# Preparing the decays of a gated linear attention anew: lines of 16 with carries, three full head groups, earlier start, unrolled tiles

## The chip, the cores and the metric

The kernel runs on one core of a Trainium2 chip. The metric is the device time of one execution in microseconds (us), median of the timed runs. The engines are TensorE (PE), VectorE (DVE), ScalarE (ACT), GpSimd (POOL) and SyncE (SP), which here only issues DMAs.

## The reference, cut to what matters

Three layers follow each other: an attention with complex decays, a SoLU expert layer, and a top-2 mixture of 8 experts. The change touches only how the decays of the first layer are prepared.

```python
# q, k, v, a_re, a_im: batch 4, heads 8, positions 768, head_dim 48
mag = np.sqrt(a_re * a_re + a_im * a_im)
scale = np.minimum(mag, 0.999) / (mag + 1e-06)
a_re_n, a_im_n = (a_re * scale, a_im * scale)
for t in range(S):
    ar, ai = (a_re_n[:, :, t, :, None], a_im_n[:, :, t, :, None])
    new_re = ar * S_re - ai * S_im
    new_im = ar * S_im + ai * S_re
    kv = np.einsum('bhd,bhe->bhde', k[:, :, t], v[:, :, t])
    S_re, S_im = (new_re + kv, new_im)
    y[:, :, t] = np.einsum('bhd,bhde->bhe', q[:, :, t], S_re)
```

Then x = y as 3072 tokens of 384; h = x @ w_in (384 to 1024); SoLU, layer norm and @ w_out (1024 to 384); router logits, top 2 of 8, and for each expert relu(x @ w1) @ w2.

## The kernel before

**Two phases.** The first phase goes over 24 tiles of 128 positions (batch b = 0..3, chunk c = 0..5, tile n = 6b + c) and ends with tokens scattered to their experts' regions in HBM. The second goes over 31 slots of 256 tokens, and the gathers write the output. The diff leaves the second phase alone, but for a renamed constant.

**Decays in a tile.** Positions of a chunk are referred to its middle. For each position the kernel holds the running complex product F of the decays from the middle outwards and 1/|F|^2. Query and key are weighed by these (`weigh`, the positions of one half each) and multiplied by F (`qp` on VectorE, `kp` on GpSimd), so that scores are plain matmuls. The state between chunks is multiplied by the "state decays" `md`.

**The preparation of a batch**, before: head pairs on 2 x 48 of the 128 partitions, 4 pairs x 6 chunks x 128 positions = 3072 elements a partition, in three pieces. Loads (`load_a`); squares (ScalarE), `m2` (GpSimd), four ScalarE passes `logs`, `zsum` (GpSimd), `scale` (ScalarE), normalising (`norm` on GpSimd, `norm_im` on VectorE), `neg` (ScalarE). Then `products_start` and the running product, `product_op`: 63 steps of three VectorE instructions of 96 elements, one position outwards on both sides of all 24 middles at a time. Then `state_decays` (8 small ones), squares, `f2`, Ln and Exp, `newton` (GpSimd), `inverses` (VectorE), and `publish` (ScalarE copies F to a second buffer). In batch 0 all this is ahead of the tiles. Batch b + 1 is prepared inside batch b: the product steps in chunks 2, 3 and 4, as `fill()` between other VectorE work; squares and logs in chunks 0 and 1, the inverse in 5.

**The tiles are software-pipelined.** In iteration n each engine works on m = n - 1 (attention), i = n - 2 (first matmul, SoLU), j = n - 3 (second matmul) and g_ = n - 4 (router), in an order written out by hand; semaphores tie the engines. TensorE: transposes of kp(m) (L1247), first half of the hidden matmuls (i) (L1285, waits for xl), score matmuls (m) interleaved with the second half (L1305, wait for qp and zl), the state product w(m) with the second matmul (j) (L1345, L1326), y(m) (L1359, L1361), logits (L1376), transposes of z(i) (L1247). y(m) goes through ScalarE's xh (L802) and VectorE's xl (L1132) to the hidden matmuls of the next iteration. VectorE's last instructions in an iteration are xl(m) and then q_products(n) (L982); GpSimd's `weigh` (L505, L507) is first and `kp` (L515) comes behind the masking of at(m) (L536), before the state products. ScalarE: zh(j) (L722), kt, wide, softplus, at(m) (L759), exp, x2, centring, x2t, xh(m). Chunks 0 to 5 of batches 0 and 3 are unrolled, batches 1 and 2 are a hardware loop whose body is six chunks.

Of the kernel before, what the change touches and what calls it, by code (L numbers as in the profile page):

```python
# [15 lines left out]
P = 128  # L16
# [7 lines left out]
F = 1024  # L24
# [11 lines left out]
PIECES = 3  # L36
CP = C // PIECES
# [38 lines left out]
def solu_moe_program(nc, q, k, v, a_re, a_im, w_in, w_out, g_ln, w_gate, w_noise, noise, w1, w2, out):  # L76
# [3 lines left out]
    with ExitStack() as ctx:  # L80
# [22 lines left out]
        ar = m1("ar", [P, NP, C, P])  # L103
        m1_ai = m1.at
        ai = m1("ai", [P, 2, NP, C, P])
        fw = m1("fw", [P, 2, NP, C, P])
        early_end = m1.at
        fu = m1("fu", [P, 2, NP, C, P])
        rc = m1("rc", [P, NP, C, P])
# [14 lines left out]
        ct1 = m1("ct1", [P, 2, G, 2])  # L124
        ct2 = m1("ct2", [P, 2, G, 2])
        hd = [m1(f"hd{i}", [P, 2, NP, C]) for i in range(3)]
        ud = [m1(f"ud{i}", [P, 2, NP, C - 1]) for i in range(2)]
        md = m1("md", [P, 3, NP, C - 1])
        mdn = m1("mdn", [P, 3, NP, C - 1])
        xh = m1("xh", [P, NP, P], F32R)  # L130
        xl = m1("xl", [P, NP, P], F32R)
        z = m1("z", [P, F])
# [56 lines left out]
        NG = 4  # L189
        m3 = Map(nc, tables_end)  # L190
        ga = [m3(f"ga{i}", [P, 2, DM]) for i in range(NG)]
        gb = [m3(f"gb{i}", [P, DM]) for i in range(NG)]
        gc = [m3(f"gc{i}", [P, DM]) for i in range(NG)]
# [10 lines left out]
        md_ready = sem("md_ready")  # L204
# [5 lines left out]
        a_re_loaded = sem("a_re_loaded")  # L210
        a_im_loaded = sem("a_im_loaded")
# [7 lines left out]
        an_re = sem("an_re")  # L219
        an_im = sem("an_im")  # L220
# [6 lines left out]
        nt_step = sem("nt_step")  # L227
        rc_done = sem("rc_done")
        pub_done = sem("pub_done")
# [58 lines left out]
        g_loaded = [sem(f"g_loaded{i}") for i in range(NG)]  # L288
        first_done = sem("first_done")
        both_done = sem("both_done")  # L290
        out_sent = [sem(f"out_sent{i}") for i in range(NG)]
# [6 lines left out]
        CUM = 4 + 3 * (HALF - 1)  # L298
        block = ctx.enter_context(nc.Block())

        def piece(t, g):
            return t[:, :, g * CP:(g + 1) * CP, :]

        def slot_piece(t, s, g):
            return t[:, s, :, g * CP:(g + 1) * CP, :]

        STEPS = {0: 0, 1: 0, 2: 19, 3: 22, 4: 22, 5: 0}
        assert sum(STEPS.values()) == HALF - 1
# [1187 lines left out]
```

## Time and profile before

| | us |
|---|---|
| timed runs, median (lowest to highest) of 3 | 1587.64 (1586.15 to 1588.35) |
| span of the profiled execution | 1599.5 |
| busy in it: TensorE / VectorE / ScalarE / GpSimd | 1197.5 / 1032.7 / 720.5 / 470.9 |
| mean granted TensorE clock | 0.890 of full speed |

The profiled execution has no time of its own beside its span, which lies 12 us above the median of the timed runs. A sum made from the profile is made against the 1599.5. The clock column of the profile is 1.0 at 2.4 GHz and 0.5 at 1.2 GHz.

### The profile page before, as it was taken

The numbers are of one execution on the slowest core, as the hardware profiler recorded it, in microseconds if no ns is written. First come the engines' busy times: TensorE is split into PE (matmuls) and PEld (weight loads), VectorE is DVE, ScalarE is ACT, GpSimd is POOL, SyncE is SP. The second block draws the span as 40 slices with busy tenths as digits, with TensorE's granted clock in tenths as the row PEclk, the third lists the DMA queues.
The fourth block names the chain that finished last, engine by engine and source line by source line (L and its number), as shares of the span: only waits on it lengthen the run. The fifth ranks groups of instructions, "written<-read, shape, count | busy, mean of one in ns | idle before, by whom it ended". The sixth has DMA issues, their size and how long they took to land.

```text
span 1599.5 us, 24940 instructions
## 1 busy us (share of the span) xinstructions
PE 1197.5 (75%) x8058; PEld 1026.0 (64%) x8058; DVE 1032.7 (65%) x2193; ACT 720.5 (45%) x1094; POOL 470.9 (29%) x378
## 2 busy tenths in 40 slices
PE   0001448888888778789999827999999999999920
PEld 0001336666666556556777627999999999999910
DVE  2896299867998569984444335666666666666523
ACT  5305622657226662254334314555555555555500
POOL 4204633467435664445345110000000000000056
PEclk9999668878888878987999958999999999999965
DMA  8103100041000401001111037666666566656357
GB/s 161 68 0 58 31 16 16 26 84 46 31 26 26 97 19 45 25 26 35 41 50 41 21 138 247 215 219 211 237 206 231 199 234 216 230 202 223 131 154 211
DMA packets 78718, 179.64 MB, mean 112 GB/s; under 512 B 7344, under 2 KB 46384, under 8 KB 77872
## 3 DMA queue, kind: packets, MB, share of 16 engines
q1 hardware_dynamic: 68032, 147.60, 29.5%
q0 software_dynamic: 6144, 18.88, 4.0%
q10 hardware_dynamic: 4464, 12.19, 1.9%
q8 instruction: 40, 0.66, 0.2%
q14 instruction: 38, 0.31, 0.1%
HBM read 146.01 MB, written 32.64 MB: 112 GB/s over the span
## 4 chain that ended last, share of the span: by engine, by line
PE 51%; DVE 20%; issue 10%; POOL 7%; DMA 5%; ACT 4%; SPq 2%; DVEq 0%; POOLq 0%; ACTq 0%
PE bank L1431 17%; PE bank L1256 16%; DVE fw L937 5%; DVE ct L934 5%; PE bank L1285 4%; PE bank L1326 4%; DVE ct L930 4%; PE bank L1247 3%; POOL ga L613 2%; DMA ai<-in_a_im 2%; PE bank L1305 2%; PE bank L1359 1%; POOL ar L489 1%; PE bank L1345 1%; POOL ai L495 1%
## 5 line engine op out<-in xcount | busy, mean ns | idle before, releaser
L613 POOL DMA_INDIRECT ga<-ys,row_u x48 | 45.9, 957 | 605.1 <-DMA ys<-yo 590.7
L1256 PE MATMUL bank<-sxh,w1h 128*128 128x256 f32 x744 | 212.3, 285 | 1.9 <-DVE sxl L1209 1.9
L1256 PE MATMUL bank<-sxh,w1l 128*128 128x256 f32 x744 | 210.3, 283 | 0.0
L1256 PE MATMUL bank<-sxl,w1h 128*128 128x256 f32 x744 | 210.2, 283 | 0.0
L858 ACT ACTIVATE hh<-bank 128x256 fp32r<-128x256 f32 x248 | 95.2, 384 | 218.7 <-PE bank L1256 218.7
L1221 DVE SCALAR_TENSOR_TENSOR hl<-bank,hh 128x256 fp32r<-128x256 f32 x248 | 104.8, 423 | 129.4 <-ACT hh L858 129.3
L1431 PE MATMUL bank<-w2h,hh 128*128 128x384 f32 x496 | 170.4, 344 | 6.1 <-DVE hl L1221 3.2
L1431 PE MATMUL bank<-w2l,hh 128*128 128x384 f32 x496 | 166.9, 336 | 0.0
L1431 PE MATMUL bank<-w2h,hl 128*128 128x384 f32 x496 | 166.7, 336 | 0.0
L1198 DVE TENSOR_TENSOR w1l<-raw,w1h 128x1024 fp32r<-128x1024 f32 x93 | 113.9, 1226 | 52.8 <-ACT w1h L822 52.8
L1247 PE MATMUL bank<-ident,kp 128*128 128x128 f32 x192 | 33.4, 333 | 151.4 <-POOL kp L515 149.7
L1256 PEld LDWEIGHTS bank<-sxh,w1h 128*128 128x128 f32 x744 | 140.8, 189 | 2.3 <-DVE sxl L1209 2.3
L1256 PEld LDWEIGHTS bank<-sxh,w1l 128*128 128x128 f32 x744 | 141.8, 191 | 0.0
L1256 PEld LDWEIGHTS bank<-sxl,w1h 128*128 128x128 f32 x744 | 141.3, 190 | 0.0
L1204 DVE TENSOR_TENSOR w2l<-raw,w2h 128x768 fp32r<-128x768 f32 x124 | 118.6, 958 | 30.9 <-ACT w2h L827 30.9
L1247 PEld LDWEIGHTS bank<-ident,kp 128*128 128x128 f32 x192 | 29.6, 177 | 151.8 <-issue 151.8
L930 DVE TENSOR_TENSOR ct<-fw,ar 128x96 f32<-128x96 f32 x252 | 104.1, 413 | 7.6
L822 ACT ACTIVATE w1h<-raw 128x1024 fp32r<-128x1024 f32 x93 | 97.7, 1052 | 19.7 <-DMA raw<-in_w 19.7
L827 ACT ACTIVATE w2h<-raw 128x768 fp32r<-128x768 f32 x124 | 103.6, 838 | 3.2 <-DMA raw<-in_w 3.2
L1431 PEld LDWEIGHTS bank<-w2h,hh 128*128 128x128 f32 x496 | 94.3, 190 | 12.1 <-issue 8.4
L934 DVE TENSOR_TENSOR ct<-fw,ai 128x96 f32<-128x96 f32 x252 | 101.1, 401 | 0.0
L937 DVE TENSOR_TENSOR fw<-ct,ct 128x96 f32<-128x96 f32 x252 | 93.6, 372 | 6.8
(182 smaller groups left out, 2920.1 us busy)
## 6 DMA issues: line engine op xcount, KB each, us to landing
raw<-in_w SPq DMA_DIRECT2D x62, 1536.0 KB, 6.7
xg<-xs SPq DMA_DIRECT2D x31, 384.0 KB, 7.1
ys<-yo ACTq DMA_DIRECT2D x31, 384.0 KB, 6.4
ar<-in_a_re SPq DMA_DIRECT2D x8, 576.0 KB, 8.2
ai<-in_a_im SPq DMA_DIRECT2D x8, 576.0 KB, 14.7
qk<-in_q SPq DMA_DIRECT2D x48, 96.0 KB
qk<-in_k SPq DMA_DIRECT2D x48, 96.0 KB
vt<-in_v SPq DMA_DIRECT2D x24, 192.0 KB, 2.4
```

Source lines behind the costliest of these rows:

```text
L822: nc.scalar.activation(w1h[par][:, cc, :], raw1[:, cc, :], ACT.Copy).then_inc(w1_hi, 1)
L827: nc.scalar.activation(w2h[par][:, W2C * j:W2C * (j + 1), :], raw2[:, W2C * j:W2C * (j + 1), :], ACT.Copy).then_inc(w2_hi, 1)
L858: nc.scalar.activation(hh[:, f % NH, :], bank[:, f % 2, 0:CAP], ACT.Relu).then_inc(hh_done, 1)
L930: V.tensor_tensor(ct1[:], fwg[:, :, :, prev], arg[:, :, :, step].to_broadcast([P, 2, G, 2]), ALU.mult).then_inc(cum_step, 1)
L934: V.tensor_tensor(ct2[:], fwg[:, ::-1, :, prev], aig[:, :, :, step], ALU.mult).then_inc(cum_step, 1)
L937: V.tensor_tensor(fwg[:, :, :, new], ct1[:], ct2[:], ALU.add).then_inc(cum_step, 1)
L1198: V.tensor_tensor(w1l[par][:, cc, :], raw1[:, cc, :], w1h[par][:, cc, :].bitcast(F32), ALU.subtract).then_inc(w1_lo, 1)
L1204: V.tensor_tensor(w2l[par][:, cut, :], raw2[:, cut, :], w2h[par][:, cut, :].bitcast(F32), ALU.subtract).then_inc(w2_lo, 1)
L1221: V.scalar_tensor_tensor(out=hl[:, f % NH, :], in0=bank[:, f % 2, 0:CAP], scalar=0.0, in1=hh[:, f % NH, :].bitcast(F32), op0=ALU.max, op1= ...
L1247: ins = nc.tensor.transpose(out_, in_, ident[:])
L1256: ins = MM(dst, stationary[a_](cc), moving[b_](cc), start=(n_ == 0), stop=(n_ == len(terms) - 1))
L1431: ins = MM(bank[:, 2 + u, 0:DM], a_[:, f % NH, rows], b_[par][:, f, :], start=(f == 0 and k_ == 0), stop=(f == FC - 1 and k_ == 2))
```

## The change

- **Layout.** The eight heads of 48 rows are packed into three groups that fill all 128 partitions (`by_lane` on the host): six heads as before, the other two, in strips of 16 rows, in the 16 rows that each pair left free. A partition has 2304 elements. The first half of each chunk is stored in reversed order. After the products, SyncE copies the strips to a fourth group (`spread_cum` 12 DMAs, `spread_md` 6, `spread_rc` 6 for each range).
- **Products.** Lines of 16 positions at a time (15 steps of three instructions, 288 elements for a whole batch), then three carries: a line is multiplied by the last element of the line before (6 instructions of 576 elements).
- **Ranges.** Batch 0 is prepared in two ranges, chunks 0 and 1 ahead of the tiles, chunks 2 to 5 behind VectorE's work of tiles 0 and 1. The others are one range each, in two parts. `PREP` says in which chunk what stands; the load of a batch can start once `newton` of the batch before has ended.
- **Engines.** `weigh` goes from GpSimd to VectorE, into q_products, behind xl. `norm` and `newton` go to VectorE, the second as two fused instructions. qp and kp become two instructions each, one for each half. `publish` goes; F has two buffers by batch.
- **Order of the start.** No memsets ahead of the first load; the low parts of the weights (`weights_rest`) are made after the query product of tile 0.
- **Unrolling.** All 24 tiles and the four that drain the pipeline are unrolled.

```diff
+RANGES = ((0, 0, 2), (0, 2, C), (1, 0, C), (2, 0, C), (3, 0, C))
+PARTS = ((0, 0, 0, 2), (1, 0, 2, 4), (1, 0, 4, 6), (2, 1, 0, 3), (2, 1, 3, 6),
+         (3, 2, 0, 3), (3, 2, 3, 6), (4, 3, 0, 3), (4, 3, 3, 6))
...
+        PREP = {0: {"load": 2, "logs": 2, "scale": 3, "chain": (4, 5), "decays": 5, "early": None, "late": 5, "post": 5}}
+        for b_ in range(1, B - 1):
+            PREP[b_] = {"load": 0, "logs": 0, "scale": 1, "chain": (2, 3, 4), "decays": 4, "early": 5, "late": None, "post": 5}
...
-            for c in range(C):
-                body(0, c, c, True)
-            with eng.Fori(1, B - 1) as b:
-                for c in range(C):
-                    body(b, c, b * C + c, True)
-            for c in range(C):
-                body(B - 1, c, (B - 1) * C + c, False)
+            for n in range(T):
+                body(n // C, n % C, n, n < T - C)
```

GpSimd (its `k_products`, and what leaves its list):

```diff
-                nc.gpsimd.tensor_tensor(qk[:, 0, :, 0:HALF], qk[:, 0, :, 0:HALF], rc[:, :, c, 0:HALF],
-                                        ALU.mult).then_inc(qkw_done, 1)
-                nc.gpsimd.tensor_tensor(qk[:, 1, :, HALF:P], qk[:, 1, :, HALF:P], rc[:, :, c, HALF:P],
-                                        ALU.mult).then_inc(qkw_done, 1)
...
-                wait(pool, pub_done, PIECES * b + c // CP + 1)
+                pool.wait_ge(qkw_done, 2 * (n + 1))
                 wait(pool, a_mm, n)
...
+                for h_ in range(2):
+                    cols = slice(HALF * h_, HALF * (h_ + 1))
+                    cum = cums[b % 2][:, :, :, 1, c, :] if h_ else cums[b % 2][:, :, :, 0, c, ::-1]
+                    nc.gpsimd.tensor_tensor(kp[:, :, :, cols], cum, qk[:, 1:2, :, cols].to_broadcast([P, 2, NP, HALF]),
+                                            ALU.mult).then_inc(kp_done, 1)
```

SyncE, in the body of a tile:

```diff
+                if when(b, c, "load"):
+                    load_a(b + 2)
...
+                if when(b, c, "decays"):
+                    spread_cum(b + 2)
+                    spread_md(b + 2)
+                if more and c == 5:
+                    spread_rc(b + 2)
```

ScalarE, in the body of a tile: the first three stand before at(m), `scale` of the second part behind exp, the rest behind xh(m).

```diff
+                if when(b, c, "logs"):
+                    act.wait_ge(w_ready, 2)
+                    act.wait_ge(gaps_ready, 6)
+                    squares(2 * b + 3)
+                    squares(2 * b + 4)
+                if when(b, c, "scale"):
+                    logs(2 * b + 4)
+                    scale(2 * b + 3)
+                if when(b, c, "early"):
+                    inverse_squares(2 * b + 3)
+                    inverse_squares(2 * b + 4)
...
+                if when(b, c, "logs"):
+                    logs(2 * b + 3)
+                if when(b, c, "scale"):
+                    neg(2 * b + 3)
+                    neg(2 * b + 4)
+                if when(b, c, "late"):
+                    inverse_squares(2 * b + 3)
+                    inverse_squares(2 * b + 4)
+                if when(b, c, "post"):
+                    inverse(2 * b + 3)
+                    inverse(2 * b + 4)
```

VectorE:

```diff
+                if k < CHAIN:
+                    v, step = k // 3 + 1, k % 3
...
+                    if step == 0:
+                        dve.wait_ge(cum_step, at0)
+                        V.tensor_tensor(t1, cum[:, :, :, :, v - 1],
+                                        blocks(ar, r)[:, :, :, v].unsqueeze(1).to_broadcast([P, 2, 2 * NG, nu]),
+                                        ALU.mult).then_inc(cum_step, 1)
...
+            def q_products(b, c, n):
+                r = b + 1 if n >= 2 else 0
+                dve.wait_ge(qk_loaded, 64 * (n + 1))
+                dve.wait_ge(rc_spread, 96 * (r + 1))
+                dve.wait_ge(rc_done, PARTS_UPTO[r])
+                V.tensor_tensor(qk[:, 0, :, 0:HALF], qk[:, 0, :, 0:HALF], rc[:, :, 0, c, ::-1], ALU.mult).then_inc(qkw_done, 1)
+                V.tensor_tensor(qk[:, 1, :, HALF:P], qk[:, 1, :, HALF:P], rc[:, :, 1, c, :], ALU.mult).then_inc(qkw_done, 1)
...
                 if has(n):
                     q_products(b, c, n)
+                if when(b, c, "scale"):
+                    norm(2 * b + 3)
+                    norm(2 * b + 4)
+                if when(b, c, "decays"):
+                    state_decays(b + 2)
+                if when(b, c, "post"):
+                    f2(2 * b + 3)
+                    f2(2 * b + 4)
+                    newton(2 * b + 3)
+                    newton(2 * b + 4)
+                if n == 0:
+                    weights_rest(0)
+                    weights_rest(1)
+                    norm(1)
+                    norm(2)
+                    products_start(1)
+                    for k_ in range(CHAIN):
+                        product_op(1, k_)
```

TensorE waits for w_ready before the first hidden matmul instead of ahead of everything; its order is the same.

## Rows read from the trace of the kernel before

**Rows 1.** Page: busy time of each engine (span 1599.5 us); the chain by engine.

```profile
PE 1197.5 (75%) x8058; PEld 1026.0 (64%) x8058; DVE 1032.7 (65%) x2193; ACT 720.5 (45%) x1094; POOL 470.9 (29%) x378
...
PE 51%; DVE 20%; issue 10%; POOL 7%; DMA 5%; ACT 4%; SPq 2%; DVEq 0%; POOLq 0%; ACTq 0%
```

**Rows 2.** Stages: start:end length, busy us (instructions) by engine, granted clock, DMA share, GB/s.

```profile
0.00:145.60 145.60, 0.00 (x0) 0.00 (x0) 102.50 (x228) 50.96 (x48) 42.52 (x31) 1.00 0.29 63
...
180.80:230.90 50.10, 20.12 (x136) 14.93 (x136) 38.83 (x76) 24.86 (x34) 26.14 (x17) 0.66 0.04 12
...
323.40:358.30 34.90, 28.07 (x164) 20.05 (x162) 20.47 (x36) 21.31 (x27) 22.10 (x17) 0.76 0.48 96
358.30:391.70 33.40, 28.90 (x188) 22.27 (x186) 22.10 (x37) 26.95 (x37) 24.22 (x14) 0.89 0.11 31
391.70:427.05 35.35, 28.60 (x170) 21.15 (x171) 33.51 (x95) 10.92 (x20) 18.80 (x17) 0.81 0.11 34
427.05:461.40 34.35, 27.41 (x175) 20.56 (x174) 32.99 (x100) 9.09 (x17) 12.58 (x12) 0.85 0.09 30
...
521.40:555.60 34.20, 27.49 (x177) 19.85 (x178) 19.63 (x37) 21.40 (x27) 22.63 (x16) 0.85 0.51 99
...
724.90:760.00 35.10, 32.67 (x165) 23.35 (x165) 13.70 (x37) 14.53 (x19) 18.27 (x16) 0.66 0.12 40
760.00:877.30 117.30, 117.30 (x867) 86.88 (x866) 56.39 (x162) 45.08 (x80) 53.61 (x53) 1.00 0.13 41
```

**Rows 3.** Timeline (start us, length us), boundary of tile 19, and one wait at 329.

```profile
329.81 1.23 PE L1305 MATMUL bank<-qp,kp 64*128 64x128 f32 x8 [3.30 <-DVE zl L1024]
...
781.73 0.43 PE L1361 MATMUL bank<-at,vt 128*48 128x128 f32 x4
782.20 0.60 ACT L802 ACTIVATE xh<-bank 112x512 fp32r<-112x512 f32 x1 [0.85 <-PE bank L1361]
782.83 0.69 DVE L1132 TENSOR_TENSOR xl<-bank,xh 112x512 fp32r<-112x512 f32 x1 [1.64 <-ACT xh L802]
783.44 1.22 DVE L982 TENSOR_TENSOR qp<-fu,qk 128x1024 f32<-128x1024 f32 x1
783.68 1.04 PE L1247 MATMUL bank<-ident,kp 128*128 128x128 f32 x8
```

**Rows 4.** Windows of TensorE alone in a chain tile: length, busy, clock.

```profile
447.20:452.10 4.90, 0.00 (x0) 0.90 0.00 0
...
454.20:461.30 7.10, 5.87 (x30) 0.50 0.09 31
```

**Rows 5.** Timeline of VectorE: a full-size product, and product steps.

```profile
50.35 3.48 DVE L962 TENSOR_TENSOR ai<-ai,fw 128x1024 f32<-128x1024 f32 x3
...
56.79 0.35 DVE L930 TENSOR_TENSOR ct<-fw,ar 128x96 f32<-128x96 f32 x1
57.05 0.35 DVE L934 TENSOR_TENSOR ct<-fw,ai 128x96 f32<-128x96 f32 x1
...
57.79 0.35 DVE L930 TENSOR_TENSOR ct<-fw,ar 128x96 f32<-128x96 f32 x1
```

**Rows 6.** GpSimd's kp beside a VectorE product (timeline); a ScalarE pass (groups).

```profile
439.60 2.46 POOL L515 TENSOR_TENSOR kp<-fu,qk 128x1024 f32<-128x1024 f32 x1
439.73 2.53 DVE L934 TENSOR_TENSOR ct<-fw,ai 128x96 f32<-128x96 f32 x1
...
L641 ACT ACTIVATE fw<-fw 128x1024 f32<-128x1024 f32 x12 | 12.7, 1059 | 0.4
```

**Rows 7.** Loads: the start, the decays of batch 1, expert weights (page).

```profile
39.35 11.08 DVE L896 TENSOR_SCALAR raw_out<-raw_out,g_sb 128x384 f32<-128x384 f32 x8 [27.52 <-DMA nz<-in_noise]
...
145.88 0.80 SPq L363 DMA_DIRECT2D ar<-in_a_re  x2
162.75 1.06 ACT L631 ACTIVATE fw<-ai 128x1024 f32<-128x1024 f32 x1 [3.92 <-DMA ai<-in_a_im]
...
raw<-in_w SPq DMA_DIRECT2D x62, 1536.0 KB, 6.7
```

More of the change, by code:

```diff
@@ L529, in body @@
-                filling = static and n == 1
-                if more and c == 1 and not filling:
-                    zsum(b + 1, 0)
-                    zsum(b + 1, 1)
+                has = lambda t: 0 <= t < T
                 if has(m):
@@ L688, in _, with neg @@
[L688 to L697 removed]
+            def neg(q):
+                act.wait_ge(an_done, 3 * (q + 1))
+                nc.scalar.activation(part(an, q), part(ai, q), ACT.Copy, scale=-1.0).then_inc(neg_done, 1)
@@ L699, in _ @@
+            act.wait_ge(tiny_ready, 2)
+            squares(0)
+            logs(0)
+            scale(0)
+            neg(0)
+            for q in (1, 2):
+                squares(q)
+            for q in (1, 2):
+                logs(q)
+            for q in (1, 2):
+                scale(q)
             act.wait_ge(raw_loaded, 48)
@@ L702, in _ @@
             nc.scalar.activation(wo_hi[:], raw_out[:], ACT.Copy).then_inc(w_hi_ready, 1)
[L703 to L709 removed]
+            inverse_squares(0)
+            inverse(0)
+            for q in (1, 2):
+                neg(q)
             def body(b, c, n, more):
[L712 removed]
                 m, i, j, g_ = n - 1, n - 2, n - 3, n - 4
[L714 to L718 removed]
+                has = lambda t: 0 <= t < T
                 if has(j):
@@ L792, in body @@
                                          accum_out=mv[c % 2][:, 2:3]).then_inc(var_done, 1)
-                if more and c == 1 and not filling:
-                    prepare(b, (scale, 0), (scale, 1), (scale, 2))
                 if has(j):
@@ new lines, in norm @@
+            def norm(q):
+                _, _, c0, c1 = PARTS[q]
+                s_ = cum_part(q, 0)
+                dve.wait_ge(sc_done, q + 1)
+                V.tensor_tensor(part(ar, q), part(ar, q), s_, ALU.mult).then_inc(an_done, 1)
+                halves = [t.rearrange("p (g h) x -> p g h x", h=2) for t in (part(ai, q), s_)]
+                low, high = ([t[:, :, h_, :] for t in halves] for h_ in range(2))
+                V.scalar_tensor_tensor(out=low[0], in0=low[0], scalar=-1.0, in1=low[1], op0=ALU.mult,
+                                       op1=ALU.mult).then_inc(an_done, 1)
+                V.tensor_tensor(high[0], high[0], high[1], ALU.mult).then_inc(an_done, 1)
@@ L1001, in body @@
                 m, i, j, g_ = n - 1, n - 2, n - 3, n - 4
-                has = lambda t: not static or 0 <= t < T
-                made = [3 * sum(STEPS[x] for x in range(c))]
-                share = made[0] + 3 * STEPS[c] if more else made[0]
+                has = lambda t: 0 <= t < T
+                chain = PREP[b]["chain"] if more else ()
+                total = CHAIN + CARRY
+                upto = lambda k: total * k // len(chain)
+                made, share = ([upto(chain.index(c))], upto(chain.index(c) + 1)) if c in chain else ([0], 0)
@@ L1058, in body @@
                     V.tensor_tensor(hot[:, 2, :], hot[:, 0, :], hot[:, 1, :], ALU.add).then_inc(gate_step, 1)
-                if more and c == 5:
-                    for g in range(PIECES):
-                        f2(b + 1, g)
-                filling = static and n == 1
-                fill(share - 20 - made[0])
+                fill(share - 8 - made[0])
                 if has(i):
@@ L1125, in body @@
                 fill(share - made[0])
-                if more and c == 1 and not filling:
-                    for g in range(PIECES):
-                        norm_im(b + 1, g)
                 if has(m):
```

628 lines of the change are left out of this document (308 added, 320 removed).

## The prediction

> **What bounds the kernel now.** I read the header and the chain first, then the span cut into stages, then the instructions at one tile boundary, and last the durations. The header and the chain [rows 1] say that TensorE is busy 75% of 1599.5 us and carries half of the chain; VectorE has 20% of it. Where each holds is read from the stages [rows 2]. I cut the first phase at q(n), the start of the query product (L982) of tile n; "body c" is the stretch that ends at the q of chunk c of its batch. Four regimes are to be seen. Until q(0) at 145.6 us TensorE does nothing and VectorE is busy for 102.5 us: the decays of batch 0 are a serial preparation. Tiles 0 and 1 are slow too (q(2) at 230.9). In the batches that prepare the next one a tile takes 33 to 39 us, and in the chain tiles (427.05 to 461.40) VectorE is busy for 33.0 of 34.35 us, so VectorE sets them. In batch 3, with nothing left to prepare, five tiles take 117.3 us, 23.46 each, with TensorE busy all the time at the full clock: that is TensorE's floor. There VectorE is busy for only 11.3 us a tile. The expert slots and the gathers behind them are the same code in both kernels; I leave them alone.
>
> **The change, part by part: the element work.** The prices of VectorE come from two rows [rows 5]: instructions of 96 elements follow each other at 0.26 us, and three of 1024 take 3.48, so one of n elements costs about 0.17 us + 0.97 ns x n, and a step of three with its two waits (1.00 us for 96 elements) costs 0.22 us above three times that. Before, a batch has 63 steps, 63 us. After, it has 15 steps of 288-element instructions, 3 x 0.45 + 0.22 = 1.56 us each, 23.4 in all, and 3 carries of six 576-element instructions, 6 x 0.73 + 0.22 = 4.6 us each, 13.8 in all: 37 us instead of 63. VectorE also gets scaling (5.4 us a batch), f2 2.6, Newton 5.1 and, in every tile, two weighings of 256 elements (0.83 us). Its sum per batch falls, and the chain tiles need 11.3 + 0.8 + 10.9 (seven steps) = 23 us, or 27.5 for the one with the carries. VectorE is no longer the bound there. What goes away on ScalarE (publish, three-part neg) and GpSimd (weigh, norm, Newton) is off the path once these engines have idle time; their share of VectorE's blocking is in the 23 us already.
> The row shows instructions of 96 elements at 0.26 us [rows 5]. The Trainium skill, VectorE: DVE Perf Modes, section The TRN2 errata, has 58 + n cycles in its table, 0.16 us for 96 elements, and says itself that the measured fixed part is nearer 150 cycles. By the table the preparation of batch 0 would be some 11 us shorter still, and my time 11 us lower; the trace agrees with the 150.
>
> **The start.** VectorE's first long wait ends when the last small load lands, at 39.35 [rows 7]. Only a third of the decays (0.8 instead of 2.4 MB) is ahead of it now: 28 us (26 to 33). Scaling w_out, norm, neg and start: 36. Chain of 96 elements, 15 x 1.00 = 15, with the four GpSimd sums of parts 1 and 2 in its way (7 us): 58. Carries 3 x 2.3: 65. Decays, squares, f2, logarithm and exponential, Newton, all serial: 71.5. Then SyncE issues 24 spreading DMAs at 0.4 us each [rows 7], most of them while that goes on, and the last land about 78: q(0), against 145.6. Behind it VectorE does in program order weights_rest 7.8, norm 4, start 1.2 and 15 steps of 192 elements (19.2), plus GpSimd's products: q(1) at 119.5, against 180.8. After that the carries, decays, f2 and Newton of the second range run until 145.5; only then may the load of batch 1 start. A pair of such loads takes 16.9 us from issue to landing [rows 7]; in rows of 128 partitions it may do as well as a weight load (1.5 MB in 6.7 us), so 10 to 16. ScalarE waits for both loads before it evacuates at(1), and q(2) follows y(1): 174, against 230.9. So the start gains 57 us.
>
> **What a tile costs then.** At a floor boundary [rows 3] y ends at 782.16, xh runs to 782.80, xl starts at 782.83, the query product at 783.44, and TensorE starts the transposes of kp at 783.68 with no wait, because GpSimd had made kp in the middle of the tile. After the change VectorE weighs q and k itself, and does so behind xl. GpSimd's kp can start only then, and TensorE's next instruction in order is the transpose of kp. From 783.44: 0.83 for the weighings, then two halves of kp (2.46 us for the whole, so 1.2 each) and two halves of the query product (0.65 each) that exclude each other: a VectorE product of 0.35 us lasts 2.53 while kp runs [rows 6]. kp is ready 3.3 (GpSimd first) to 4.5 us after TensorE wants it. Behind kp in GpSimd's queue stand the state products, the scatter and rstd; their readers (wide about 8 us into the tile, x2 about 20) come later. The load of the next q and k waits for kp too, and has 20 us of cover. Nothing is charged for these. So TensorE gets a gap of 3.3 to 4.5 us in every tile, and the floor becomes 23.46 + 4.0 = 27.5. The clock comes on top: in the 4.9 us gap from 447.20 the granted clock falls, and it is 0.50, the 1.2 GHz level, until 461.30 [rows 4]: 9.1 us at half speed behind the gap, in which at most 4.5 us of work are lost. Bounds 0 and 4.5; the work behind the new gap is denser than there, so I take the middle, 2.5, and 30 us a tile; with the gap's own bounds a tile lies between 26.8 and 32.5.
> The Trainium skill, TensorE: Matmul & The Clock Gate, section HAM oscillation, speaks against this change in the same way: a wait repeated in each iteration lets each one start at the lower clock. By full clock throughout, the five last tiles would give back 12 us of what I charge.
>
> **The preparation around the boundaries.** ScalarE's zh of the next tile stands behind the preparation of this one, and zl and the score products wait for it; one such wait of 3.30 us is there already [rows 3]. Its instructions of 1024 elements take 1.06 us [rows 6], those of 1152 some 1.2. Body 1: squares are summed by GpSimd only behind kp, so logs (4 x 1.25) end 11.7 us after the weighing, zl 2.2 later, and TensorE wants it at 8: 30 + 6 = 36. Body 2: norm of both parts on VectorE, interleaved with GpSimd's state products, ends at 11.8, neg at 13, then start and four fills stand ahead of zl: ready at 17.4, so 40. Bodies 3, 4, 5: 30, 31, 30. Body 0: f2, ScalarE's inverse and Newton end at 13.9, zl is 15.3; the load is issued behind the six rc spreads at 16.6, lands after 10 to 16 us, and all four squares stand ahead of at: 43 (40 to 47). Body 0 of batch 3 has no load: 37.5.
>
> **The sum**, beside before [rows 2]: bodies 3, 4, 5 of batch 0 (36, 40, 37, two chain shares of 19 us each) give q(5) at 287 against 323.4; body 0, 45: q(6) at 332 against 358.3. Batch 1: 167 and 43: q(12) at 542 against 555.6. Batch 2: 167 and 37.5: q(18) at 746.5 against 760.0. Batch 3: 5 x 30 = 150: q(23) at 896.5 against 877.3, and kp(23) is later by 4: +23. At 27.5 a tile it is +11. I take +15. The profiled execution spans 1599.5, so the changed one spans about 1614; it lies 12 above the median of the timed runs (1587.64), and on their footing the forecast is 1603. Unrolling I cost at nothing: batch 3 is unrolled before as well, and TensorE is never idle in it. The looped tiles leave VectorE idle for 1.4 us of 34.35 [rows 2], so the most that registers can cost is 12 x 1.4 = 17 us; what sets these tiles afterwards is kp, so none of it is taken.
>
> **Rivals.** (1) Faster: the stalls of zl at the boundaries do not come about, because the ScalarE and VectorE work there fits into the gap that kp opens anyway. For it: kp's gap ends 4 us into the tile and only what is later than 8 us costs. Price: 6 in body 1, 10 in body 2, 7 in body 0, three times: up to 69, likely two thirds, 46: 1603 - 46 = 1557. It decides from 15 us on, that is from a fifth of the price. (2) The gap at kp isn't there or is under 1 us (if GpSimd's halves overlapped VectorE): 9 tiles that TensorE bounds win 6 us, 54: 1549; rows 6 speak against it. (3) The start's gain is given back to the last microsecond: 1587 +- 3. (4) Worse: the loads land late as well and the clock stays low for two thirds of each tile: 20 tiles x 1.5 + 3 x 4 = 42 more, 1645. (5) The page's VectorE table holds: 1592.
>
> **Chances and range.** Slower as forecast or by (4): 0.56, of it (4) 0.08. Rival (1) 0.28, (2) 0.06, (5) and other small gains 0.04: faster 0.38. Within 0.2% (3 us, about what a measurement can tell from no change): 0.06. The range 1560 to 1635 leaves out the upper part of (4) and the lower parts of (1) and (2). The likeliest case's own range is 1592 to 1625.
>
> **What would show it.** Right: q(0) near 78, q(2) near 174; in the last five tiles of the first phase a period near 30, a wait of TensorE's kp transposes for GpSimd of 3.3 to 4.5 us in each, and a granted clock below 1 where it was 1.00; score products that wait for zl in bodies 0, 1 and 2. Wrong: a period of 24 there, or batches 1 and 2 well under 200 us, or a start that ends after 100 us.

## The result, and the profile after

| | before | after |
|---|---|---|
| timed runs, median (lowest to highest), us | 1587.99 (1586.15 to 1592.81), 4 runs | 1605.95 (1603.61 to 1606.88), 4 runs |
| span of the profiled execution | 1599.5 | 1603.5 |
| mean granted TensorE clock | 0.890 | 0.880 |

The changed kernel is slower, by 1.1%: the ratio is 1.0107, with a 95% interval of 1.0086 to 1.0129. The forecast was 1603 us and slower.

The page of the kernel after, busy time of the engines and the chain by engine, answers to [rows 1]:

```profile
PE 1203.9 (75%) x8058; PEld 1031.3 (64%) x8058; DVE 919.7 (57%) x1864; ACT 659.5 (41%) x1022; POOL 380.3 (24%) x316
...
PE 53%; issue 18%; DVE 9%; POOL 7%; SPq 4%; ACT 4%; DMA 3%; POOLq 0%; ACTq 0%; DVEq 0%
```

VectorE lost 113 us of work and fell from 20% to 9% of the chain; GpSimd lost 91, ScalarE 61. The time did not follow. The windows of the kernel after, cut at q(n) like [rows 2] and with the same columns, say where it stayed:

```profile
0.00:73.40 73.40, 0.00 (x0) 0.00 (x0) 40.55 (x102) 28.70 (x29) 15.69 (x23) 1.00 0.48 129
112.82:165.47 52.65, 21.41 (x136) 15.64 (x136) 25.82 (x46) 17.16 (x22) 10.18 (x6) 0.61 0.21 68
277.24:321.18 43.94, 32.27 (x181) 23.27 (x179) 22.58 (x51) 20.68 (x27) 12.21 (x10) 0.74 0.32 97
321.18:359.17 37.99, 31.10 (x173) 22.69 (x173) 9.99 (x36) 20.48 (x26) 17.80 (x11) 0.78 0.08 26
359.17:394.55 35.38, 25.58 (x173) 18.95 (x173) 30.67 (x71) 11.80 (x19) 16.61 (x10) 0.86 0.10 29
...
424.46:454.83 30.37, 25.97 (x173) 19.24 (x173) 26.77 (x58) 9.37 (x17) 13.19 (x10) 0.89 0.11 33
485.23:523.79 38.56, 28.66 (x173) 20.73 (x173) 20.39 (x42) 18.01 (x24) 16.66 (x10) 0.82 0.29 95
686.49:722.85 36.36, 26.93 (x173) 19.85 (x173) 20.38 (x43) 13.90 (x21) 16.65 (x10) 0.86 0.14 36
722.85:872.24 149.39, 129.64 (x865) 96.09 (x865) 49.52 (x177) 45.76 (x81) 47.18 (x47) 0.91 0.11 35
```

The last row is the clearest. Five tiles of batch 3, which prepare nothing, took 117.30 us at the full clock in [rows 2]; now they take 149.39 with the same matmuls. By stages, from these rows and the starts of the query product that lie between them:

| stretch | before | after | difference |
|---|---|---|---|
| to q(2) | 230.9 | 165.5 | -65.4 |
| q(2) to q(5) | 91.6 | 111.8 | +20.2 |
| q(5) to q(11) | 198.9 | 208.0 | +9.1 |
| q(11) to q(17) | 203.5 | 201.3 | -2.3 |
| q(17) to q(18) | 35.0 | 36.4 | +1.3 |
| q(18) to q(23) | 117.3 | 149.4 | +32.1 |
| behind q(23) | 722.2 | 731.3 | +9.0 |

They sum to +4.0, the difference of the two spans; the medians differ by 18.0. The last of the experiments shows where the other 14 are. The timeline of the kernel after at the last tile boundary (start us, length us) answers to [rows 3]:

```profile
870.34 0.60 ACT L802 ACTIVATE xh<-bank 112x512 fp32r<-112x512 f32 x1 [0.85 <-PE bank L1413]
870.40 0.35 SPq L427 DMA_DIRECT2D vt<-in_v  x1
870.91 1.07 PE L1300 MATMUL bank<-ident,z 128*128 128x128 f32 x8
870.96 0.69 DVE L1172 TENSOR_TENSOR xl<-bank,xh 112x512 fp32r<-112x512 f32 x1 [3.16 <-ACT xh L802]
871.57 0.41 DVE L1030 TENSOR_TENSOR qk<-qk,rc 128x256 f32<-128x256 f32 x1
871.90 0.42 DVE L1031 TENSOR_TENSOR qk<-qk,rc 128x256 f32<-128x256 f32 x1
...
872.24 1.28 DVE L1038 TENSOR_TENSOR qp<-cum,qk 128x512 f32<-128x512 f32 x2
872.41 3.47 POOL L557 TENSOR_TENSOR kp<-cum,qk 128x512 f32<-128x512 f32 x2 [11.95 <-DVE qk L1031]
...
875.93 0.90 PE L1300 MATMUL bank<-ident,kp 128*128 128x128 f32 x3 [3.95 <-POOL kp L557]
```

Read upwards from the last row: TensorE has done the transposes of z and then idles 3.95 us for kp; kp began 0.09 us after the second weighing ended; the weighing stands behind xl; and GpSimd had idled for 11.95 us before it. The data was there, only the order was not. The view of waits (TensorE, 60 to 900 us; total, times, longest) says it for all tiles:

```profile
PE bank L1300 <- POOL kp L557: 214.7, 24, 88.4
PE bank L1411 <- POOL at L575: 24.7, 3, 20.8
PE bank L1357 <- DVE zl L1076: 23.4, 8, 6.6
```

The longest, 88.4, is the start, and so are the 19.1 us of the tile after it. The other 22 are one in each tile, 107.2 us together. They are not equally long: 3.95 where nothing is prepared, 6.5 in bodies 0 of batches 2 and 3, and 9.16 in bodies 2. The timeline of the boundary into body 2 of batch 1 (GpSimd's kp, VectorE's normalising, TensorE):

```profile
359.34 8.69 POOL L557 TENSOR_TENSOR kp<-cum,qk 128x512 f32<-128x512 f32 x2 [9.31 <-DVE qk L1031]
...
360.38 1.35 DVE L1002 TENSOR_TENSOR ar<-ar,cum 128x1152 f32<-128x1152 f32 x1
...
364.92 0.75 DVE L1007 TENSOR_TENSOR turn_a<-turn_a,cum 128x576 f32<-128x576 f32 x1
...
368.08 1.97 PE L1300 MATMUL bank<-ident,kp 128*128 128x128 f32 x8 [9.16 <-POOL kp L557]
```

VectorE's products stand back to back from 359.17 to 365.67, 6.5 us, at their usual pace; kp takes 2.50 us in the middle of a tile of the kernel with early weighing (below), and 8.69 here, about the sum of both. GpSimd gets only what VectorE leaves here.

### The profile page after: what moved, and what is told of

It is laid out like the page before. It is cut to its first block, busy times and chain, and to the rows that moved or that the text cites. A ratio compares the mean times of both kernels' runs of the same rounds, so it can differ in the third digit from the quotient of the medians.

```text
span 1603.5 us, 23562 instructions
## 1 busy us (share of the span) xinstructions
PE 1203.9 (75%) x8058; PEld 1031.3 (64%) x8058; DVE 919.7 (57%) x1864; ACT 659.5 (41%) x1022; POOL 380.3 (24%) x316
## 3 DMA queue, kind: packets, MB, share of 16 engines
q1 hardware_dynamic: 75424, 151.17, 28.9%
## 4 chain that ended last, share of the span: by engine, by line
PE 53%; issue 18%; DVE 9%; POOL 7%; SPq 4%; ACT 4%; DMA 3%; POOLq 0%; ACTq 0%; DVEq 0%
PE bank L1483 17%; PE bank L1309 16%; PE bank L1336 8%; PE bank L1357 3%; PE bank L1300 3%; POOL ga L647 3%; PE bank L1378 2%; POOL kp L557 2%; DMA turn_a<-in_a_im 2%; SPq L395 1%; POOL at L575 1%; PE bank L1411 1%; ACT at L765 1%; DVE ct L939 1%; DVE cum L949 1%
## 5 line engine op out<-in xcount | busy, mean ns | idle before, releaser
L1300 PE MATMUL bank<-ident,kp 128*128 128x128 f32 x192 | 46.8, 425 | 214.7 <-POOL kp L557 214.7
L1300 PEld LDWEIGHTS bank<-ident,kp 128*128 128x128 f32 x192 | 37.3, 222 | 220.4 <-POOL kp L557 132.1
L557 POOL TENSOR_TENSOR kp<-cum,qk 128x512 f32<-128x512 f32 x48 | 110.1, 2313 | 265.4 <-DVE qk L1031 265.4
L1336 PE MATMUL bank<-wi_hi,xh 112*128 112x512 f32 x192 | 99.6, 519 | 0.0
L1357 PEld LDWEIGHTS bank<-qp,kp 64*128 64x128 f32 x768 | 57.4, 208 | 60.3 <-issue 60.3
```

The lines of the kernel that those rows point to most:

```text
L557: nc.gpsimd.tensor_tensor(kp[:, :, :, cols], cum, qk[:, 1:2, :, cols].to_broadcast([P, 2, NP, HALF]), ALU.mult).then_inc(kp_done, 1)
L1300: ins = nc.tensor.transpose(out_, in_, ident[:])
L1336: ins = MM(bank[:, 4 + half, :], (xh, xl)[a_][0:PR, cc, :], (wi_hi, wi_lo)[b_][0:PR, cc, 512 * half:512 * half + 512], start=(k_ % (3 * NP ...
L1357: ins = MM(bank[:, 2 + h_, p_ * P:(p_ + 1) * P], kp[r_, s, p_, :], qp[r_, s, p_, :], start=(s == 0), stop=(s == 1))
```

## The experiments

Where q(n) is given for a kernel, it is the start of its query product. "The kernel before" in each ratio was timed on the same chip. My theory: the wait for kp, made by weighing behind xl, costs each tile its gap and then a stretch at the lower clock. Rivals: the half-size products or something else in the new code is slow wherever it stands; the preparation at the boundaries is what counts; the gap is dear only because TensorE has nothing else in it.

**Weighing earlier.** VectorE weighs q and k of the next tile in the middle of this one, ahead of the maximum for the SoLU, instead of behind xl; GpSimd also waits for the copied strips.

```diff
+                if has(n):
+                    weigh(b, c, n)
...
                 if has(n):
                     q_products(b, c, n)
```

> The changed kernel with the weighing of q and k moved in VectorE's order from behind xl to the middle of the tile (ahead of nmax), so that GpSimd makes kp behind the mask of at, as before the change. Theory A (kp, chained behind xl, is what lengthens every tile): the 3.95 us gap of TensorE at the kp transposes is gone, the five last tiles take 23.7 us instead of 29.9 with the clock at 1.00, the tiles of chunks 3 to 5 in batches 1 and 2 some 25.5 instead of 30.4, body 0 and 1 some 2 to 3 us less each; in all about 95 us less than the changed kernel: 1511 us. Rival B (the preparation work at the boundaries and VectorE's fuller list set the tiles, and kp only waits where something else is late anyway): under 30 us less, 1576 or more, and the last tiles stay above 28.

Measured: 1499.11 us (1493.78 to 1507.95), ratio 0.9432 (0.9368 to 0.9496), 107 us below the changed kernel and 12 below what I expected. The windows of the first body of batch 3 and of the five tiles after it:

```profile
616.18:658.82 42.64, 34.96 (x175) 25.19 (x174) 17.54 (x42) 13.56 (x20) 10.71 (x10) 0.64 0.12 36
658.82:775.92 117.10, 117.10 (x867) 86.67 (x866) 57.92 (x176) 45.07 (x80) 47.37 (x48) 1.00 0.13 41
```

The five tiles are back at the floor, 23.42 each, so the half-size kp costs nothing where it isn't waited for. Two rows of this kernel's timeline at such a boundary, beside the 3.95 us above:

```profile
728.42 1.07 PE L1307 MATMUL bank<-ident,z 128*128 128x128 f32 x8
...
729.33 1.04 PE L1307 MATMUL bank<-ident,kp 128*128 128x128 f32 x8
```

It is the one position of two instructions that turns a kernel 1% slower than before into one 5.7% faster. What is left above the floor is now in the waits for zl:

```profile
PE bank L1364 <- DVE zl L1081: 56.4, 13, 8.5
```

They were 23.4 in 8 before the edit: part of what kp's wait had covered now shows itself, in bodies 0 (37.9 to 42.6 us) and 2 (34.7 and 34.9). Body 0 of batch 3, 36.4 us before the edit, even takes 42.6, at a clock of 0.64; body 0 of batch 2 has the same wait of 7.68 us and takes 37.9 at 0.82.

**The wait alone, in the kernel before.** GpSimd's kp waits for xl in all chunks but 1; nothing else of the change is in.

```diff
+                if c != 1:
+                    apart(pool, (xt_lo, n))
```

> The kernel before the change with one wait more: GpSimd's kp of a tile waits for xl of the tile before (in chunks 0, 2, 3, 4, 5; in chunk 1 it would deadlock). Its decays, layout and loops are those of before. Theory A: TensorE gets a gap of 3.0 to 3.6 us at the kp transposes and the lower clock behind it: the five last tiles go from 23.5 to about 29 but for chunk 1, the chain tiles stay at 34 to 36 (VectorE sets them), the tiles of chunk 5 go from 25.7 to about 30; in all some 60 us more than before: 1648 us. Rival B: under 20 us more.

Measured: 1675.82 us (1663.58 to 1679.95), ratio 1.0552 (1.0495 to 1.0609). In batch 3 its tiles are 28.3, 23.5 (the one left alone), 29.5, 28.3 and 29.6 us. The tile left alone, the one behind it, and TensorE's wait in the latter:

```profile
821.22:844.68 23.46, 23.46 (x175) 17.37 (x174) 9.68 (x33) 9.02 (x16) 4.27 (x6) 1.00 0.11 35
844.68:874.22 29.54, 26.47 (x175) 19.62 (x174) 9.87 (x34) 9.15 (x16) 10.84 (x11) 0.88 0.11 35
...
848.15 1.97 PE L1249 MATMUL bank<-ident,kp 128*128 128x128 f32 x8 [3.07 <-POOL kp L517]
```

So the gap of 3.1 us and 1.7 to 3.1 behind it are there in this kernel too, with no other part of the change. Over the whole kernel it is 28 dearer than I expected, mostly in bodies 0 and 1 of batches 1 and 2: they take 33.4 to 39.1 us in the profile of before and 40.7 to 47.2 here, where waits for zl of 2.2 to 7.2 us come on top.

**Filling the gap.** From tile 1 on, TensorE issues 14 matmuls of constants ahead of the transposes of kp.

```diff
+                    if m >= 1:
+                        pe.wait_ge(w_ready, 2)
+                        for _ in range(14):
+                            MM(bank[:, 0, :], wi_hi[0:PR, 0, 0:P], wi_hi[0:PR, 1, 0:512], start=True, stop=True)
                     pe.wait_ge(kp_done, 2 * (m + 1))
```

> The changed kernel with fourteen matmuls on constant weights, whose results are overwritten, ahead of TensorE's wait for kp from tile 1 on; they fill about 3.3 of the 3.95 us and depend on nothing. This separates the clock from the wait. Theory A (of the 6.4 us that a last tile takes above 23.5, 3.95 are the wait and 2.5 the lower clock behind it): last tiles 27.5 with the clock at 1.00, in all about 40 us less than the changed kernel: 1565 us. Rival C (the clock costs nothing, the rest is later lateness): last tiles stay at 29 to 30 and the time at 1606 or a little above.

Measured: 1587.63 us (1575.38 to 1598.36), ratio 0.9991 (0.9955 to 1.0027). The last five tiles:

```profile
720.12:858.46 138.34, 134.42 (x936) 99.50 (x936) 49.51 (x176) 46.16 (x81) 47.33 (x47) 1.00 0.12 38
```

That is 27.67 each at the full clock, against 29.88 at 0.91: kp's wait takes its full length, and of the 6.4 us above the floor 2.2 are the clock. Matmuls that compute nothing give 18 us. I had expected 40: bodies 0, 1 and 2, whose length a longer wait for kp or zl sets, fell by at most 1.4 us. Body 0 of batch 3 takes 44.9 us at a clock of 0.66 in this execution, against 36.4 at 0.86 in the changed kernel's; that is 8.5 us of what is missing.

**Other work ahead of kp's transposes.** TensorE does the first 12 hidden matmuls first, and the transposes of kp behind them.

> The changed kernel with one edit in TensorE's order: the first twelve hidden matmuls, which need only xl, stand ahead of the transposes of kp. Nothing on VectorE or GpSimd changes. Theory A (it is the gap in TensorE's own order that costs): the twelve matmuls take 2.8 of the 3.95 us, 1.2 are left, the clock stays up, last tiles near 25, in all about 75 us less than the changed kernel: 1530 us. Rival B (kp's lateness costs through what reads it later: kt, w, the state): last tiles stay near 29 and the time above 1585.

Measured: 1612.92 us (1601.89 to 1626.86). The profiled execution is the longest of the four, 1626.86; the median of the other three is 1603.81, and the ratio, taken without it, 1.0125 (1.0044 to 1.0205). So only its tiles that wait for nothing else are read closely:

```profile
774.00:898.30 124.30, 118.33 (x866) 86.72 (x866) 49.51 (x176) 46.12 (x81) 47.23 (x47) 1.00 0.13 42
```

These fall from 29.9 to 24.9 as expected, 25 us in all, and yet the kernel gains nothing. In bodies 1 of batches 1 and 2 the two waits, 3.95 or 3.67 us for kp and 2.95 or 3.51 for zl, have become one of 8.56 or 8.55 for zl, with 1.2 left for kp in batch 1; body 2 still has two, 6.38 and 4.25. In this execution bodies 1 and 2 of batch 1 take 44.1 and 46.7 us at clocks of 0.65 and 0.60, and the waits for zl sum to 80.7 in 15. I expected 1530 and missed by 83, or by 74 without the longest execution. The gap at kp was not pure loss in these bodies, since zl was late anyway; and the clock there is lower than in the changed kernel (0.78 and 0.86). In batch 2 of the same execution these bodies take 36.1 and 37.7 us at 0.86 and 0.82, against 36.0 and 35.4 in the changed kernel: there the order alone gives neither gain nor much loss. Why the clock in batch 1 is lower, the run doesn't tell.

**The preparation one chunk later.** On top of the early weighing, in batches 1 and 2.

```diff
-            PREP[b_] = {"load": 0, "logs": 0, "scale": 1, "chain": (2, 3, 4), "decays": 4, "early": 5, "late": None, "post": 5}
+            PREP[b_] = {"load": 0, "logs": 1, "scale": 2, "chain": (3, 4, 5), "decays": 5, "early": None, "late": 5, "post": 5}
```

> The kernel with early weighing (1499 us), with the whole preparation of the next batch one chunk later in batches 1 and 2: squares and logs in chunk 1, normalising in 2, products in 3 to 5, inverse in 5. Nothing is left out. Theory (what is left above the floor is preparation that ScalarE and VectorE do in program order ahead of what TensorE wants next, and the load of the decays that ScalarE waits for ahead of at(m)): body 0 no longer waits for the load, 38 to about 32 us in two batches, body 1 gets it instead but the load has landed, 24 to about 33, body 2 takes what body 1 had, 35 both: about 0 to -10 us, 1490 to 1499, with the stall moved from body 0 to body 1. Rival (the load was the larger part of the stall in body 0): -10 to -20, about 1484. Rival 2 (late squares and the inverse at the end of chunk 5 make the next body 0 longer): 1505.

Measured: 1509.77 us (1495.07 to 1515.20), ratio 0.9466 (0.9388 to 0.9544). Body 0 falls from 42.6 and 37.9 to 35.2 and 35.1 us, as the load theory has it, and body 2 of batch 1 from 34.9 to 28.9 (in batch 2 it takes 35.9, at a clock of 0.67); body 3 rises from 25.7 to 34.2. The stall has moved with the normalising, to body 3 and not to body 1 as I had expected. The waits for zl are the same:

```profile
PE bank L1364 <- DVE zl L1081: 58.1, 14, 8.7
```

The median is 11 above that of the kernel with early weighing, and the intervals of the two ratios overlap, so neither a gain nor a loss is shown. In the profiled executions q(5) to q(18) is 6.0 us shorter, while batch 0, which the edit leaves alone, takes 12.7 more up to q(5).

**The preparation behind zh and zl.** Also on top of the early weighing: ScalarE's logs, neg and inverse and VectorE's normalising, state decays, f2, Newton and start of products stand behind zh(j) and zl(j) of the next iteration. With them go GpSimd's zsum and the product steps ahead of zl, and in chunk 0 the weighing stands behind the SoLU block.

```diff
-                if when(b, c, "scale"):
-                    norm(2 * b + 3)
-                    norm(2 * b + 4)
...
+                if left(n, "scale"):
+                    norm(2 * pb + 3)
+                    norm(2 * pb + 4)
```

> The kernel with early weighing (1499 us), with the preparation that stands behind xh(m) on ScalarE (logs, neg, inverse) and behind the query product on VectorE (normalising, state decays, f2, Newton, start of products) moved behind zh and zl of the next tile; nothing is left out. Theory (the score matmuls wait for zl, because ScalarE and VectorE first do this preparation; those waits sum to 56 us in the kernel with early weighing): most of them go, bodies 2 from 35 to about 28 and bodies 0 from 38 to 33, some 8 us a batch in three batches and twice that in batch 0: 1460 to 1475. Rival (the same work then delays at(m) or the SoLU block of the same tile, which TensorE wants a few us later, and the load starts later by as much): 1490 to 1500.

Measured: 1518.88 us (1515.54 to 1519.52), ratio 0.9538 (0.9484 to 0.9592), 20 slower than without the edit by the medians and 17 by the ratios. Both my theory and the size of the rival were wrong. One row of the waits tells why nothing was won:

```profile
PE bank L1384 <- DVE hot L1126: 56.8, 13, 9.0
```

The waits for zl, 56.4 us in 13, are gone, and TensorE waits 56.8 us in 13 for the one-hot masks of the router instead, which VectorE makes next. Bodies 2, 3 and 4 of batch 1 take 39.2, 30.1 and 31.7 us against 34.9, 25.7 and 26.8. The waits in them are hardly longer than before (9.0 for 8.5 us in body 2); the clock is lower, 0.74, 0.77 and 0.78 against 0.85, 1.00 and 0.99. Body 3, with the early weighing alone and then with this edit:

```profile
363.94:389.63 25.69, 23.63 (x176) 17.43 (x175) 25.05 (x58) 9.13 (x16) 10.48 (x11) 1.00 0.13 39
```

```profile
369.97:400.08 30.11, 29.26 (x175) 21.16 (x174) 24.98 (x58) 9.24 (x16) 9.55 (x10) 0.77 0.11 33
```

TensorE is idle for only 0.85 us in the second, and its matmuls take 5.6 us longer. The six bodies 2 to 4 of batches 1 and 2 are 27 us longer together, more than the whole loss; why the clock is lower there, no run shows.

**Both of these together.**

> Both of the two edits above together: preparation one chunk later, and behind zh and zl. Nothing is left out. Theory: the two gains add, as they lie at different places (load ahead of at(m), and zl): 1450 to 1465. Rival (the stalls only move to the next consumer): 1485 to 1500, and the granted clock stays near 0.91.

Measured: 1516.78 us (1513.62 to 1522.29), ratio 0.9534 (0.9474 to 0.9593). Body 2 of batch 1 is down to 24.2 us and body 3 up to 38.9; the wait for the masks is 65.7 in 13. The rival's mechanism held, 17 us past its range, and the granted clock is 0.878, not its 0.91. None of the three placements tried hides the block of some 6 us of preparation: each time a result was due behind it.

**Filling the waits for zl.** Early weighing, and in five bodies (0 of batches 1 to 3, 2 of batches 1 and 2) 16 to 32 matmuls of constants in the wait for zl.

```diff
+                    for _ in range({6: 16, 8: 32, 12: 28, 14: 32, 18: 28}.get(n, 0)):
+                        MM(bank[:, 5, :], wi_hi[0:PR, 0, 0:P], wi_hi[0:PR, 1, 0:512], start=True, stop=True)
```

> The kernel with early weighing (1499 us), and in five tiles in which TensorE waits 4.6 to 8.5 us for zl, the first body of each batch after batch 0 and body 2 of batches 1 and 2, 16 to 32 matmuls of constants of 0.23 us each are issued in that wait, into a bank that the next hidden matmul overwrites. Nothing is left out. Theory (a long wait costs twice: itself, and the work done behind it at the 1.2 GHz level, above all in the first body of batch 3, where the clock is low for 30.7 us): the waits stay, the low stretches behind them go; that body falls from 42.6 to about 29, the two first bodies of batches 1 and 2 by 2 and 5, the two bodies 2 by 3 each: 1475, q(5) to q(18) shorter by 20 to 26. Rival (the waits alone set these tiles, because what follows waits for VectorE and not for TensorE): 1495 to 1500, the first body of batch 3 then at 36 to 43.

Measured: 1494.04 us (1493.14 to 1511.57), ratio 0.9429 (0.9362 to 0.9497); by the medians 5 us less than without, inside the spread of either. The first body of batch 3:

```profile
616.27:647.45 31.18, 29.96 (x203) 22.67 (x202) 17.55 (x42) 13.47 (x20) 10.74 (x10) 1.00 0.17 49
647.45:765.02 117.57, 117.57 (x867) 87.05 (x866) 57.90 (x177) 45.08 (x80) 47.52 (x48) 1.00 0.13 41
```

42.6 us have become 31.2, where the theory had 29. How much of that the filler gives in general is not shown: the 42.6 are of one execution at a low clock, and the medians differ by 5. Bodies 0 of batches 1 and 2 stayed at 42.1 and 37.9, as the rival said. In batch 2 ScalarE waits 8.7 and 2.6 us for the two loads, does its four squares, and has at(m) only 27.6 us into the tile; TensorE then waits 3.1 us for it. In batch 1 the waits are longer still, 12.8 and 1.4, and 4.5 for at(m). Bodies 2 fell by less than 2, though their clock rose from 0.85 to 1.00. Of the 20 to 26 us that I expected between q(5) and q(18), the profiled executions have 15.4, and 11.5 of these are that one body. The median, 1494, lies next to the rival's 1495 to 1500 and far from the theory's 1475.

**Unrolling alone**, in the kernel before.

```diff
-            with eng.Fori(1, B - 1) as b:
+            for b in range(1, B - 1):
```

> The kernel before, with its hardware loop over batches 1 and 2 written out, as one part of the change alone; nothing else differs and nothing is left out. Theory (unrolling gains nothing, because what sets a looped tile is a wait of TensorE or VectorE's products, not its registers): within 0.3% of before, tiles of batches 1 and 2 at 33 to 35 us as looped. Rival (registers and branches take up to VectorE's idle 1.4 us in a tile): up to 17 us less, about 1573.

Measured: 1586.73 us (1584.72 to 1595.36), ratio 0.9978 (0.9952 to 1.0003). Chain tiles take 34.2 us written out, against 34.3 looped. No gain can be told from none.

**The kernel before, profiled once more.**

> The kernel before, unchanged, profiled once more. Its first profile spans 1599.5 us, 12 above the median of its timed runs, with a granted clock of 0.890. If the spread between executions (1583 to 1601) is the granted clock's, this profile near 1585 to 1590 has a clock near 0.90 and the same instructions' durations otherwise, and the last five tiles still take 117.3 us. If instead profiling itself costs about 12 us, the span is again near 1599.

Measured: 1587.50 us (1583.00 to 1596.52), the profiled execution 1587.88 with a span of 1586.1. Profiling doesn't cost 12 us; the first profile had caught a long execution. Its body 0 of batch 3, which took 35.10 us at a clock of 0.66 in [rows 2], and the five tiles behind it:

```profile
719.88:745.54 25.66, 22.60 (x163) 16.40 (x164) 13.57 (x37) 14.44 (x19) 18.29 (x16) 1.00 0.17 55
745.54:862.87 117.33, 117.33 (x867) 86.90 (x866) 55.46 (x162) 45.10 (x80) 53.63 (x53) 1.00 0.14 41
```

That one tile is 9.4 of the 13.4 us between the two spans: the same instructions, once at 0.66 and once at the full clock. Against this profile the changed kernel's span is +17.4, which is what the medians say. In the table of stages q(17) to q(18) is then +10.7 instead of +1.3; the five last tiles are +32.1 as before.

## Why the prediction was right, and what in it was not

**The verdict and its mechanism** were right. TensorE waits 3.95 us for kp in each of the last five tiles (forecast 3.3 to 4.5), and the clock costs 2.2 more, forecast 2.5: 29.88 a tile for a forecast of 30. The trace settles the bounds: neither the 27.5 of full clock nor 32.5. Weighing early takes all of it away, and the wait alone brings most of it into the kernel before. The Trainium skill, TensorE: Matmul & The Clock Gate, section HAM oscillation, has a wait repeated in each iteration let each one start at the lower clock. These runs agree: the last tiles run at 0.91 with the wait empty and at 1.00 with matmuls of constants in it.

**The sum by its own terms.** The forecast had q(23) at 896.5 and it came at 872.2, 24.3 earlier; what is behind q(23) was forecast at 726.2 and took 731.3.

- The start was sized 8.5 us too long at q(2) (174 for 165.5). The first range is ready at 62.2, not 71.5: the last small load lands at 23.8 instead of 28, scaling and normalising take 6 us instead of 8, the 15 steps 20.5 instead of 22, and the carries 5.6 instead of 7. The spreading DMAs give some of it back: VectorE waits 10.5 us for them, where I had 6.5.
- Bodies 3 to 5 of batch 0: 111.8 for 113; the first body behind them 43.9 for 45.
- Bodies 1 and 2: 38.0 and 35.4 for 36 and 40 in batch 1. In body 2 the step that failed is "norm of both parts on VectorE, interleaved with GpSimd's state products, ends at 11.8". The norm isn't slowed and ends 6.5 us into the tile. It is GpSimd's kp that is held up by it, and kp's wait there is 9.16 us where I had 3.3 to 4.5; zl, ready at 15.1 instead of 17.4, then costs only 0.6 more. Body 0 has the same with f2, a wait of 6.5 us. I had the victim of the contention wrong, and with it the name of the wait; my length was 4.6 us too long. Bodies 1 to 5 come to 164.1 and 162.7 us for 167 each.
- Body 0 of batch 2: 38.6 for 43. The load of the next decays is issued behind the rc spreads 17.2 us into the tile, as forecast (16.6), but ScalarE has its first half 6.8 us later and all four squares done by 515, when I had allowed 10 to 16 us for landing.
- Body 0 of batch 3: 36.4 for 37.5. The last five tiles: 149.4 for 150.
- Behind q(23): +9.0 on the first profile where I had +4. Up to the first slot it takes 93.2 instead of 86: the 3.95 us wait, and a clock of 0.73 instead of 0.76 in the transition, which I had not charged.

These sum to 24.2 early in the first phase and 5.1 late behind it: 19 less than the 1622.5 of the sum at 30 us a tile, and 10.5 less than the 1614 that I took. Those 1614 had no sum of their own: I went from +23 to +15 because 27.5 us a tile would give +11. But that +11 lowers the last five tiles alone; bodies 3 to 5 of batches 1 and 2, charged at 30 and 31 too, would fall by another 15 us or more. So that lower bound was too high, and the +15 is a choice and not a result.

**Why the forecast in us was nevertheless within 3 of the median.** I subtracted 12 to get from the profile to the timed runs. That is right for the profile of before, where 9.4 of it is one body at the lower clock, but the terms of the change were partly differences against that unlucky body and its neighbours. So two errors, too long a sum and a footing that belongs to one execution, met the change's real +18 at my +15, and this is luck. The nearness of 1603 to 1606 is worth less than the 29.88 for 30.

**The rivals.** (1), that the zl stalls don't come about, fell: they come in bodies 0 and 1 (2.9 to 6.6 us), with only 0.6 in body 2 where kp's wait is long, and are 23.4 us beside kp's wait, 56.4 without it. Bodies 0, 1 and 2 of batches 1 and 2 and body 0 of batch 3 stand 54 us above 30 us each, for 68 in my sum. Later placement of the preparation only changed the name of the wait. (2), no gap at kp, fell: two halves of kp take 3.47 us together beside the query product, and the wait is 3.95. (3), within 3 us of no change, fell with +18. (4) fell: a mean of 0.91 in the last five tiles is the 1.2 GHz level for 18% of them and not for two thirds. (5) fell: a product step of three instructions of 96 elements takes 0.95 us at the start, against 1.00 in [rows 5]. The first range was ready 9.3 us earlier than I had it, but only 1.5 of that are the product steps. Unrolling at nothing held.

**What stays open.** The clock of single bodies differs between executions of the same program, by up to 9.4 us for one body, and no run shows what decides it. Most readings of single bodies rest on one profiled execution of each kernel, so differences of some us in one body may be of this kind; the five last tiles of batch 3, equal to 0.1 us in both profiles of the kernel before, are not. A repeat of the early-weighed kernels long enough to tell 1494 from 1499 was not made.

## What to carry to other kernels

When work moves from an idle engine to a busy one, look not at its length but at where in the order of the new engine it stands, and who wants the result first: 0.75 us of weighing behind xl cost 107 us that the same instructions half a tile earlier did not. When a change relieves the bound of one kind of stage, multiply what it adds by the number of tiles of every kind: here it gave 65 us once, at the start, and took 6.4 in each of the last five tiles, which VectorE had never bounded. And before a sum is carried from a profile to timed runs, see in which rows the profiled execution is longer than the others.

## What the runs showed of the hardware that was not expected

- VectorE's and GpSimd's products exclude each other, and here it is GpSimd that waits; in [rows 6] it was VectorE, so which of them does seems to hang on who comes first and runs on without a pause. kp's two halves (2.50 us together in the middle of a tile, with early weighing) take 3.47 us beside 1.28 us of VectorE products, 6.02 beside 3.9 (body 0 of batch 2), and 8.69 beside 6.5: in each case nearly the sum. Hence, for the same shape, a mean of 1.43 us a half with early weighing and of 2.31 in the changed kernel. The boundary into body 0 of batch 2 in the changed kernel, and the groups of both kernels (busy us, mean ns of one, then idle before), the changed one first:

```profile
485.23 1.29 DVE L1038 TENSOR_TENSOR qp<-cum,qk 128x512 f32<-128x512 f32 x2
485.39 6.02 POOL L557 TENSOR_TENSOR kp<-cum,qk 128x512 f32<-128x512 f32 x2 [11.95 <-DVE qk L1031]
486.43 2.62 DVE L1012 TENSOR_TENSOR turn_a<-ar,turn_a 128x1152 f32<-128x1152 f32 x2
```

```profile
L557 POOL TENSOR_TENSOR kp<-cum,qk 128x512 f32<-128x512 f32 x48 | 110.1, 2313 | 265.4 <-DVE qk L1031 265.4
```

```profile
L558 POOL TENSOR_TENSOR kp<-cum,qk 128x512 f32<-128x512 f32 x48 | 67.7, 1431 | 25.1 <-DVE qk L1032 25.1
```

The Trainium skill, SBUF — State Buffer, section Who interferes with whom, has the two engines share a pair of ports under an exclusive lock; these rows agree with it.
- In a wait of 7.68 us in the first body of batch 3 the clock fell to the 1.2 GHz level, 3.8 us before the wait ended, and stayed there for 30.7 us, though TensorE was busy for the 26.9 us behind the wait. The window of that stretch, in the kernel with early weighing:

```profile
624.09:654.81 30.72, 26.88 (x116) 18.85 (x116) 10.22 (x34) 6.83 (x13) 4.63 (x4) 0.50 0.05 10
```

With matmuls of constants in the wait the same body ran at 1.00 throughout. In and behind a wait of the same 7.68 us in body 0 of batch 2, in the same execution, the clock was low for 13.7 us and not for 30.7:

```profile
450.00:463.70 13.70, 10.10 (x42) 6.93 (x44) 6.05 (x17) 3.08 (x6) 0.00 (x0) 0.50 0.52 179
```

What makes the difference, no run shows.
